# Routing two groups of tiles at a time, behind a ring of ten row tiles, in a fused attention and mixture-of-experts kernel

## The reference

```python
# attention: a gated linear recurrence, batch 4, 8 heads, 768 steps, head width 48
f = 1 / (1 + exp(-f_logit))
for t in range(S):
    state = f[:, :, t, :, None] * state + einsum('bhd,bhe->bhde', k[:, :, t], v[:, :, t])
    y[:, :, t] = einsum('bhd,bhde->bhe', q[:, :, t], state)
x = y, laid out as 3072 tokens x 384

# mixture of 8 experts, one expert per token
logits = x @ w_gate + modality_bias[modality_id]
e_idx = argmax(logits, axis=1)
out[e_idx == e] = gate_w * (relu(x[e_idx == e] @ w1[e]) @ w2[e])     # gate_w: the softmax weight of e_idx

# gated dense layer
xn = rms_norm(x) * rms_g
out = (silu(xn @ w_gate2) * (xn @ w_val)) @ w_out
```

## Time and profile before

| | us |
|---|---|
| median of 3 runs | 860.37 (860.11 to 860.67) |
| the profiled execution | 857.94 |
| its span, first to last instruction | 856.2 |
| attention, from the span's start to its last logits | 149.5 |
| busy in the span: PE, DVE, ACT, POOL | 821.0, 471.3, 385.9, 127.4 |

### The profile page before, as it was taken

One profiled execution on the slowest core, in us unless ns is written; L12 is line 12 of the kernel. 1 busy time (PEld: TensorE's weight loads), 2 busy tenths in 40 slices (PEclk: granted clock), 3 DMA queues, 4 the chain that ended last, 5 costly groups with the idle time before them and its releaser, 6 DMA issues.

```text
span 856.2 us, 15107 instructions
## 1 busy us (share of the span) xinstructions
PE 821.0 (96%) x5300; PEld 750.8 (88%) x5300; DVE 471.3 (55%) x782; ACT 385.9 (45%) x742; POOL 127.4 (15%) x143
## 2 busy tenths in 40 slices
PE   6899997789999999989999999999999999999997
PEld 6788886779999999989888888888888888888887
DVE  8999997778767666643544343343334334333332
ACT  5888886455665555553323312331231223123112
POOL 3012113248444000010000200100020010001001
PEclk9999999999999999999999999999999999999999
DMA  9877756698987787732000100200020000000000
GB/s 190 175 157 181 169 133 240 224 364 251 306 257 244 263 319 268 243 98 71 22 1 14 61 1 1 73 0 0 0 73 0 0 37 0 0 0 37 0 0 37
DMA packets 44086, 96.54 MB, mean 113 GB/s; under 512 B 9168, under 2 KB 25040, under 8 KB 43920
## 3 DMA queue, kind: packets, MB, share of 16 engines
q1 hardware_dynamic: 39952, 85.81, 34.2%
q0 software_dynamic: 3840, 9.47, 3.1%
q10 hardware_dynamic: 256, 0.79, 0.3%
HBM read 76.75 MB, written 19.29 MB: 112 GB/s over the span
## 4 chain that ended last, share of the span: by engine, by line
PE 78%; issue 2%; DVE 1%; DMA 1%; SPq 0%; POOL 0%; ACT 0%; DVEq 0%; ACTq 0%
PE h_ps L1771 16%; PE h_ps L1773 16%; PE h_ps L1772 16%; PE ym_ps L1771 7%; PE ym_ps L1773 7%; PE ym_ps L1772 7%; PE xTm_ps L1772 3%; PE xTm_ps L1771 3%; PE xTm_ps L1773 3%; PE xT_ps L1788 1%; PE xTm_ps L1779 1%; DMA w_in<-in_w 1%; POOL out L1434 0%; ACT w_hi L1452 0%; SPq L1292 0%
## 5 line engine op out<-in xcount | busy, mean ns | idle before, releaser
L1746 DVE TENSOR_TENSOR gs<-h_ps,sig 128x512 f32<-128x512 f32 x72 | 49.8, 691 | 176.2 <-ACT sig L1546 176.2
L1546 ACT ACTIVATE sig<-h_ps 128x512 f32<-128x512 f32 x72 | 43.1, 598 | 159.5 <-PE h_ps L1773 159.5
L1557 ACT CAST h_hi<-hid 128x512 fp32r<-128x512 f32 x72 | 44.6, 620 | 149.6 <-DVE hid L1749 149.6
L1771 PE MATMUL h_ps<-x_hi,w_hi 128*128 128x256 f32 x312 | 89.3, 286 | 7.2 <-DVEq L1673 3.8
L1773 PE MATMUL h_ps<-x_lo,w_hi 128*128 128x256 f32 x312 | 89.2, 286 | 0.0
L1772 PE MATMUL h_ps<-x_hi,w_lo 128*128 128x256 f32 x312 | 89.0, 285 | 0.0
L1771 PE MATMUL h_ps<-w_hi,wg_hi 128*128 128x512 f32 x216 | 85.5, 396 | 0.0
L1773 PE MATMUL h_ps<-w_lo,wg_hi 128*128 128x512 f32 x216 | 84.6, 392 | 0.0
L1773 PE MATMUL h_ps<-w_lo,wv_hi 128*128 128x512 f32 x216 | 84.2, 390 | 0.0
L1771 PE MATMUL h_ps<-w_hi,wv_hi 128*128 128x512 f32 x216 | 84.0, 389 | 0.0
L1772 PE MATMUL h_ps<-w_hi,wv_lo 128*128 128x512 f32 x216 | 84.0, 389 | 0.0
(11 more groups left out here) (231 smaller groups left out, 1831.1 us busy)
## 6 DMA issues: line engine op xcount, KB each, us to landing
w_raw<-in_w SPq DMA_DIRECT2D x52, 384.0 KB, 5.1
w_in<-in_w SPq DMA_DIRECT2D x52, 384.0 KB, 5.4
qkf_in<-in_qkf SPq DMA_DIRECT2D x43, 288.0 KB, 5.0
y_sorted<-x_group SPq DMA_DIRECT2D x13, 384.0 KB, 3.4
v_in<-in_v SPq DMA_DIRECT2D x24, 192.0 KB, 4.6
x_regions<-zero_row SPq DMA_DIRECT2D x12, 384.0 KB, 3.4
x_group<-x_regions SPq DMA_DIRECT2D x12, 384.0 KB, 3.9
g_in<-in_wg SPq DMA_DIRECT2D x3, 768.0 KB, 7.7
```

Of the source, the lines that this page charges most:

```text
L1546: nc.scalar.activation(sig[:], g_ps, ACT.Sigmoid).then_inc(sig_done, 1)
L1557: nc.scalar.copy(h2_hi[:, fb % HELD], hid[:]).then_inc(h2_hi_done, 1)
L1746: nc.vector.tensor_tensor(gs[:], g_ps, sig[:], ALU.mult).then_inc(gs_done, 1)
L1771: nc.tensor.matmul(out, hi, rhs_hi, start=first, stop=False)
```

## The change

It does six things, all but the last in `attention`:

1. `choose`, `count` and `place` take a width w, in tiles. They run three times: tiles 0 to 7, 8 to 15 and 16 to 19 (`BATCHES`), in the places where chunks 1, 3 and 4 were handled (choose in steps 10, 18, 22; count and place in steps 12, 20, 24). The last chunk is handled in the expert stage as before.
2. x becomes a ring of ten tiles (`SLOTS`): tile n is copied to slot n % 10 and waits for the scatter of tile n-10.
3. GpSimd issues the scatters of a batch in a row. Those of tiles 4 to 11 still wait until tile n+6 has been kept; the others wait for nothing but the row numbers. Tiles 12 to 15 count on a semaphore of their own.
4. The five operations of the token bias move from DVE to GpSimd, after GpSimd's other constants.
5. The memset of `grown` moves from DVE to GpSimd, ahead of its wait for the two first clamps; that of yT_ps goes behind the first two scans. SP's small loads (gate weights, modality, bias) wait for five constants instead of seven; DVE's wait before the steps is for four. PE's warm-up has 20 products instead of 22.
6. `ks`, `state` and `grown` are 112 columns wide instead of 128; the later stages use the new slots of x.

```diff
-    def choose(self, nc, dve, c, marks, count):
+    def choose(self, nc, dve, c, w, marks, count):
...
-        tiles = bass.ds(c * B, B)
-        step(1, nc.vector.tensor_tensor(self.biased[:], self.logits[:, tiles, :], self.token_bias[:, tiles, :], ALU.add))
+        tiles = bass.ds(c * B, w)
+        biased, chosen = self.by_token(self.biased, w), self.by_expert(self.chosen, w)
+        restart = self.restart if w > B else self.restart_one
+        step(1, nc.vector.tensor_tensor(biased, self.logits[:, tiles, :], self.token_bias[:, tiles, :], ALU.add))
...
-    def scatter(self, nc, half, b, x_regions):
+    def scatter(self, nc, n, x_regions):
...
-                in_=self.x[:, half, b, :], in_offset=None)
+                in_=self.x[:, n % SLOTS, :], in_offset=None)
...
-        RT_MADE = 7
-        BIAS_STEPS = 4
+        RT_MADE = 8
+        BIASES = RT_MADE + 5
+        BATCHES = ((0, 2 * B), (2, 2 * B), (4, B))
+        LATE = 12
+        BATCH_OF = {g + w // B - 1: i for i, (g, w) in enumerate(BATCHES)}
...
-            sp.wait_ge(consts, CONSTS)
+            sp.wait_ge(consts, GATES)
...
+                pool.wait_ge(bias_landed, 32)
+                nc.gpsimd.tensor_copy(mod[:], mod64[:].bitcast(I32)[:, 0:2 * NT:2]).then_inc(rt_made, 1)
+                pool.wait_ge(rt_made, RT_MADE + 1)
+                nc.gpsimd.tensor_scalar(unmod[:], mod[:], -1.0, 1.0, ALU.mult, ALU.add).then_inc(rt_made, 1)
+                pool.wait_ge(rt_made, RT_MADE + 2)
+                nc.gpsimd.tensor_tensor(rt.token_bias[:], per_expert(bias_in[:, 0]), per_token(unmod[:]), ALU.mult).then_inc(rt_made, 1)
+                nc.gpsimd.tensor_tensor(bias1[:], per_expert(bias_in[:, 1]), per_token(mod[:]), ALU.mult).then_inc(rt_made, 1)
+                pool.wait_ge(rt_made, RT_MADE + 4)
+                nc.gpsimd.tensor_tensor(rt.token_bias[:], rt.token_bias[:], bias1[:], ALU.add).then_inc(rt_made, 1)
...
             nc.gpsimd.memset(turn_gate[:, :, 2 * D:XG], 0.0).then_inc(consts, 1)
+            nc.gpsimd.memset(grown[:], 0.0).then_inc(consts, 1)
             pool.wait_ge(f_clamped, FIRST_TWO)
...
-            def step(c, b, half):
-                if not (at(c, 0) or at(c, 1)):
-                    pool.wait_ge(marks, (c - 1) * Routing.PLACED)
-                    if not at(c, CH):
-                        pool.wait_ge(x_kept, (c - 1) * B + b + 1)
-                    pool.sem_inc(ordered, 1)
-                    rt.scatter(nc, half, b, x_regions).then_inc(ended if at(c, CH) else scattered[b], 16)
+            token_bias()
+            for i, (g0, w) in enumerate(BATCHES):
+                pool.wait_ge(marks, (i + 1) * Routing.PLACED)
+                pool.sem_inc(ordered, 1)
+                for n in range(g0 * B, g0 * B + w):
+                    if B <= n < LATE:
+                        pool.wait_ge(x_kept, n - B + SLOTS + 1)
+                        pool.sem_inc(ordered, 1)
+                    rt.scatter(nc, n, x_regions).then_inc(scattered[n % B] if n < LATE else scattered_late if n < LATE + B else ended, 16)
...
-                    slot = half if b == B - 1 else 1 - half
-                    if not (at(t[0], 0) or at(t[0], 1)):
-                        act.wait_ge(scattered[s], (t[0] - 1) * 16)
-                    nc.scalar.copy(rt.x[:, slot, s, :].rearrange("p (j r) -> p j r", j=PR),
+                    if n >= SLOTS:
+                        before = n - SLOTS
+                        if before < LATE:
+                            act.wait_ge(scattered[before % B], 16 * (before // B + 1))
+                        else:
+                            act.wait_ge(scattered_late, 16 * B)
+                    nc.scalar.copy(rt.x[:, n % SLOTS, :].rearrange("p (j r) -> p j r", j=PR),
...
-                if at(c, 0) and b == B - 1:
-                    token_bias()
...
-                if b == B - 2 and not (at(c, 0) or at(c, CH)):
+                if b == B - 2 and c - 1 in BATCH_OF:
+                    i = BATCH_OF[c - 1]
+                    g, w = BATCHES[i]
+                    if i == 0:
+                        dve.wait_ge(rt_made, BIASES)
                     dve.wait_ge(x_kept, c * B)
-                    rt.choose(nc, dve, c - 1, marks, (c - 1) * Routing.PLACED)
-                if b == 0 and not (at(c, 0) or at(c, 1)):
-                    dve.wait_ge(counted, c - 1)
-                    rt.place(nc, dve, c - 2, half, rt_ps[:, 0], rt_ps[:, 1], marks, (c - 2) * Routing.PLACED)
+                    rt.choose(nc, dve, g, w, marks, i * Routing.PLACED)
+                if b == 0 and c - 2 in BATCH_OF:
+                    i = BATCH_OF[c - 2]
+                    g, w = BATCHES[i]
+                    dve.wait_ge(counted, i + 1)
+                    rt.place(nc, dve, g, w, g * B, rt_ps[:, 0], rt_ps[:, 1], marks, i * Routing.PLACED)
...
-            nc.vector.memset(grown[:], 0.0).then_inc(filled, 1)
-            nc.vector.memset(yT_ps[:], 0.0).then_inc(yT_zero, 1)
-            dve.wait_ge(filled, 4)
+            dve.wait_ge(filled, 3)
             for b in range(FIRST_TWO):
                 sums(0, b, b)
-            dve.wait_ge(consts, CONSTS)
+            nc.vector.memset(yT_ps[:], 0.0).then_inc(filled, 1)
+            dve.wait_ge(consts, 4)
```

More of the change, by code:

```diff
@@ L47 @@
 HELD = 3
+SLOTS = 10
 RMS_EPS = 1e-6
@@ L76, in __init__, with by_expert, by_token @@
         self.before = sb("before", [P, P])
[L77 to L82, removed]
+        self.restart = sb("restart", [P, 2 * B * E])
+        self.restart_one = sb("restart_one", [P, B * E])
+        self.biased = sb("biased", [P, 2 * B * E])
+        self.most = sb("most", [P, 2 * B])
+        self.first = sb("first", [P, 2 * B])
+        self.chosen = sb("chosen", [P, E * 2 * B])
+        self.upto = sb("upto", [P, E * 2 * B])
         self.shift = sb("shift", [P, E])
-        self.rows = sb("rows", [P, E, B])
-        self.row_f = sb("row_f", [P, B])
-        self.row = [sb(f"row{h}", [P, B], U32) for h in range(2)]
+        self.rows = sb("rows", [P, E * 2 * B])
+        self.row_f = sb("row_f", [P, 2 * B])
+        self.row = sb("row_of", [P, NT], U32)
         self.chosen_all = sb("chosen_all", [P, CH, E, B])
         self.row_all = sb("row_all", [P, CH, B])
-        self.x = sb("x_group", [P, 2, B, DM])
-    def choose(self, nc, dve, c, marks, count):
+        self.x = sb("x_tiles", [P, SLOTS, DM])
+    def by_expert(self, a, w):
+        return a[:, 0:E * w].rearrange("p (e b) -> p e b", b=w)
+    def by_token(self, a, w):
+        return a[:, 0:E * w].rearrange("p (b e) -> p b e", e=E)
+    def choose(self, nc, dve, c, w, marks, count):
         def step(k, ins):
@@ L114, in choose @@
[L114 to L121, removed]
+            return a[:, 0:w].rearrange("p (b o) -> p b o", o=1).broadcast_to([P, w, E])
@@ L123, in step, with count, place @@
+    def count(self, nc, w, pre_ps, cnt_ps):
+        last = self.by_expert(self.upto, w)[:, :, w - 1]
+        nc.tensor.matmul(pre_ps, self.before[:], last, start=True, stop=True)
+        return nc.tensor.matmul(cnt_ps, self.ones_r[:], last, start=True, stop=True)
+    def place(self, nc, dve, c, w, to, pre_ps, cnt_ps, marks, count):
         def step(k, ins):
@@ L282, in attention @@
         kT = sb("kT", [P, B, PR, P])
-        ks = sb("ks", [P, B, PR, P])
+        ks = sb("ks", [P, B, PR, ROWS])
         scores = sb("scores", [P, 2, 2, PR, P])
-        state = sb("state", [P, B, PR, P])
-        grown = sb("grown", [P, B, PR, P])
+        state = sb("state", [P, B, PR, ROWS])
+        grown = sb("grown", [P, B, PR, ROWS])
         fade = sb("fade", [P, B, PR])
```

125 lines of the change are left out of this document (58 added, 67 removed).

## The result

| | before | after |
|---|---|---|
| median of 5 runs, us | 860.37 (858.0 to 861.4) | 864.98 (863.48 to 865.21) |
| the profiled execution, us | 857.94 | 864.78 |
| its span, us | 856.2 | 863.0 |
| its mean granted clock | 0.996 | 0.980 |

The ratio of the times is 1.0053, interval 1.0036 to 1.0071: slower by 4.6 us, where 859.6 and a range of 856.3 to 862.1 were forecast. In the 87 executions of the kernel before that ran beside the experiments, the mean granted clock lay between 0.979 and 0.994 and the time was the longer the lower it was: 857.4 to 858.1 us at 0.994, 861.8 to 862.5 us for all but one of those at 0.984. The profiled one, at 0.996, is above them all.

The account below looks back on a forecast made before the run. TensorE was taken to bound attention's steady steps. The terms -1.25 - 1.48 + 0.3 - 1.4 + 3.3 + 0.1 - 0.3 gave about -0.8 us, from the median 860.37 to 859.6 us; range 856.3 to 862.1.

Parts of the forecast that it names:

- Part 4: Tile 10's x copy waits for its ring slot's scatter, holding ScalarE 3.6 to 4.6 us: +3.3 us (2.9 to 3.9).
- Part 1: Two routing rounds fewer in attention: -1.95 us; two wider rounds cost +0.56 and +0.14; in sum -1.25 us.
- VectorE is the bound after all: Attention: each removed routing round is worth its 2.69 us, 3.4 us more gain: 856.2 us; chance 0.12.
- Parts 2 and 3: Token biases moved to GpSimd: -1.48 us, +0.3 for interference; earlier start after moving two memsets: -1.4 us.
- Part 4, tile 18: Step 21: tile 18's copy waits for scatter 8, but what it feeds waits for VectorE anyway: +0.1 us.
- Both waits are paid: Attention: scatter 8 lands 6 us after issue, so kT of step 22 is 2.7 us late: 862.3 us; chance 0.16.
- The ring's wait is nearly free: Tile 10's scatter lands 2.6 us after issue, TensorE about 0.4 late; 3 us come back: 856.7 us; chance 0.20.
- Part 5: Tail: TensorE's wait for x_ahead, behind the last scatter, changes by -0.3 us, within -1.0 to +1.0.

Follow-up runs that it names:

- The filled gap: The changed kernel with 14 idle products on TensorE in step 14, where it waits for the ring: 862.31 us, ratio 1.0023.
- the paced kernel: The changed kernel with twelve ring tiles, four routing rounds (8, 4, 4, 4 tiles) and scatters of tiles 4 to 7 spaced out: 857.30 us, ratio 0.9968.
- the ring of twelve: The changed kernel with twelve ring tiles instead of ten, first eight scatters in one burst: 858.91 us, ratio 0.9989; on another chip 857.61 us, 0.9974.

## Why the prediction was wrong

**The step that failed** is in Part 4: "Together 3.2 us, and 0.1 for the place that is longer: +3.3 us", followed by "Nothing gives it back". The wait itself was nearly right: ScalarE was held for 4.55 us (3.6 to 4.6 forecast), the scatter landed 5.8 us after issue, 6.8 after its row numbers (6.0 to 7.0), x of tile 11 came 3.24 us late (2.5), and with the clock kept the wait cost 3.76 us (3.3). The cost that the step put at nothing is the clock: the sum took each matmul at its length in the trace of before, all at 1.00. After 3.17 us of idling the engine ran at 0.50, and the next tile cost another 2.83 us, 2.4 of it clock; in three other profiles 1.6 us, 1.2 of it clock. The filled gap gave 2.7 us back in the median, and with the wait taken away 5.5 to 6.1 us went. The Trainium skill has the rule, in TensorE: Matmul & The Clock Gate, "HAM oscillation — how this bites in real kernels": a wait for data that leaves the array idle can put the next work at half rate. The trace agrees, and the rule belonged in the sum.

**Part 1** held: tile 4 to 5 became 1.05 us shorter and tile 12 to 13 0.91 us with the two rounds that went; the wide choose put 0.29 us before each count (0.28 forecast) and its gap from 0.41 to 0.69. TensorE bounds these steps. One sign that the prediction named did not come: kT of step 7 was to be about 4 us earlier than 45.96 and came at 44.04, because the start had given 0.78 us and not 2.6. The rival *VectorE is the bound after all* is refuted by the same rows.

**Parts 2 and 3** had the right mechanisms for the part that stands alone (2.46 of 2.58 us in one execution, 1.9 us in the median). In the changed kernel 0.78 us was left by tile 3; its clock was at 0.50 from 13 to 23 us, after the warm-up, cut to 20 products, had left TensorE idle for 2.95 us. That idle isn't the whole of it: before, 2.24 us did no harm, and in the paced kernel 2.26 did. Nor is the clock: of nine profiles with this start six had half clock in it and gained 0.8 to 1.6 us by tile 3, three kept the clock and gained 1.2, 2.1 and 2.7. The result's profile is the poorest of the nine. The contention for which the prediction cited the Trainium skill (SBUF — State Buffer, "Who interferes with whom") came as that page has it, 1.76 us for the clamp instead of 0.42. The prediction called it small because the load of tile 2 sets the time later; no run contradicts it. TensorE's first turn, which waits for VectorE's qT, came at 11.90 with the fill moved and at 12.37 to 12.46 with it in the way, but tile 3's x showed nothing of that.

**Part 4, tile 18** was right: ScalarE was held for 1.72 us at 131.68 and TensorE's idle for logits there was 2.04 us, where it had been 1.97. *Both waits are paid*, the rival that ends slower, came nearest in time and is wrong in its mechanism. *The ring's wait is nearly free* falls with the gap.

**Part 5** took -0.3 within -1.0 to +1.0. Tiles 21 to 22 lost 1.73 us and the experts 1.43. The burst was as long as estimated (10.4 us; 7 x 1.3 to 1.6 is 9.1 to 11.2) and began 4.1 us late behind the ring. What was left out is what it does to the loads beside it: those of v landed after 10.5 us instead of 8.2, a wait of 1.91 us and half clock followed. The late start of the burst did its part in that. How much this costs differs between executions: with the ring of twelve tile 21 to 22 took 4.0 us more than before in one profile and 1.3 us less in another, where the slow stretch stood three tiles earlier.

The sum by the rows: the forecast's -0.8, plus 2.8 for the ring's stage (6.06 where 3.3 was forecast; 2.3 of it clock), 1.8 for the start, 2.0 for the tail and 1.4 for the experts comes to 7.2 us; tile 22 to the experts gave 0.4 back, and measured were 6.8 between the profiles. The 2.2 us by which this exceeds the medians' 4.6 belong to the luck of the two profiled executions, which no trace divides among the stages. In the chances, the cases as listed make 0.43 faster, not 0.40.

## What to carry to other kernels

A wait on the path of a TensorE-bound stage is priced as its idle time plus the matmuls behind it at half clock; here a gap of 3.2 to 3.3 us cost 6.1 us in one profile and 5.0 in three. So look for the granted clock in every stretch that a change leaves emptier, and prefer a buffer more (here two tiles of memory) to a wait, even one of 3 us. Saving routing work of 2.7 us a round on an engine that isn't the bound gave 0.9 to 1.05 us a round, while the eight scatters that it bunched up took about 2 us in the tail: count what a burst does to the transfers beside it. That spreading the first batch gains anything is not shown.

## What the runs showed of the hardware

- A gap of 3.17 us was followed by about 6 us at 0.50 of the clock, one of 3.25 to 3.32 us at the same place in three other profiles by about 3.4 us. One of 1.91 us in the tail was followed by half clock too, one of 2.24 us in the start of the kernel before was not.
- The same idle can go either way: ahead of tile 19's x all 14 profiles have 1.94 to 2.04 us of waiting, and in 8 of them the clock fell to 0.50 there, which made tile 19 to 20 take 5.6 us or more instead of 4.3. The start of the changed kernel had half clock in 6 of 9 profiles.
- A VectorE tensor_scalar of 128x512 took 1.76 us beside a GpSimd memset of 128x1792 that had begun 0.11 us before it, 0.42 without one; it ended 0.28 us behind the memset.
- An indirect scatter landed 2.6 us after its issue in the quiet and up to 6.9 us after it beside loads or other scatters (before and after); a plain load of v among them took 10.5 us.
- The same kernel was 0.8% slower than the one before on one chip, with a stop of 4.8 us that no instruction of its core explains, and 0.2% faster on another. A gain below half a per cent has to be measured on more than one chip.
